# Gate logits summed inside attention, routing by prefix scans, one block at least for every expert

## The reference

```python
# 1: attention, q/k/v of (4, 8, 576, 64), with a learned bias on relative position
scores = q @ k.T / 8 + bias            # bias[h, i, j] from a small MLP of log distances
attn   = softmax(scores);  o = attn @ v
x = o.transpose(0, 2, 1, 3).reshape(2304, 512)        # token = batch * 576 + position
# 2: mixture of experts, top 1 of 8
logits = x @ w_gate                                    # (2304, 8)
expert_idx = argmax(logits);  gate_w = softmax(logits)[expert_idx]
for e in range(8):                                     # an expert without tokens is skipped
    out[mask] = gate_w[mask] * (relu(x[mask] @ w1[e]) @ w2[e])   # w1 512x1024, w2 1024x512
# 3: RMS norm, then silu(xn @ w_gate) * (xn @ w_val) @ w_out, 512 -> 1536 -> 512
```

## Time and profile before

| | |
|---|---|
| runs (us) | 1209.17, 1210.5, 1210.6; median 1210.5 |
| profiled execution (us) | 1211.22, its span 1209.4 |
| PE busy | 1092.7 us, 90% of the span |
| DVE, ACT, POOL busy | 733.8, 515.4, 255.9 us |
| granted PE clock, mean | 0.960 of full |
| DMA | 107.66 MB |

### The profile page before, as it was taken

The page is one execution under the profiler, slowest core; times in us unless marked ns, Lnnn a source line. Parts: engine busy times, 40 slices in busy tenths (PEclk is TensorE's granted clock), DMA queues, the critical chain, the costliest instruction groups (busy, mean ns, idle before and its releaser), DMA issues. The chain is left out here.

```text
span 1209.4 us, 23282 instructions
## 1 busy us (share of the span) xinstructions
PE 1092.7 (90%) x6540; PEld 910.2 (75%) x6541; DVE 733.8 (61%) x1310; ACT 515.4 (43%) x1047; POOL 255.9 (21%) x183
## 2 busy tenths in 40 slices
PE   3969999999996539999999947999999999999998
PEld 1347777777774338878888837999999999999997
DVE  6956656656653654282522227877778778777665
ACT  4967777777662233261522235423222232231211
POOL 3027656655600021020110115320000000000000
PEclk9989999999998759999999987999999999999999
DMA  5574644647305266182111125100010000000000
GB/s 128 231 275 95 173 101 111 171 98 204 80 25 173 97 245 214 43 286 78 35 43 43 42 97 149 60 27 26 0 52 0 26 26 0 26 26 0 27 1 27
DMA packets 71728, 107.66 MB, mean 89 GB/s; under 512 B 28176, under 2 KB 40464, under 8 KB 71696
## 3 DMA queue, kind: packets, MB, share of 16 engines
q1 hardware_dynamic: 68496, 96.78, 26.2%
q0 software_dynamic: 3200, 10.49, 2.8%
HBM read 79.85 MB, written 27.39 MB: 89 GB/s over the span
## 5 line engine op out<-in xcount | busy, mean ns | idle before, releaser
L1438 DVE RECIPROCAL f_eg<-f_eg 128x384 f32<-128x384 f32 x72 | 183.3, 2546 | 0.0
L519 DVE CUSTOM_DVE_ANT_0 a_sc<-a_s_ps,a_bias 128x576 f32<-128x576 f32 x144 | 108.3, 753 | 87.0 <-PE a_s_ps L438 73.3
L1403 ACT ACTIVATE f_eg<-f_g 128x384 f32<-128x384 f32 x72 | 35.4, 492 | 284.5 <-PE f_v L1473 284.4
L584 ACT ACTIVATE a_pr<-a_sc,a_nmax 128x576 f32<-128x576 f32 x144 | 111.9, 777 | 39.3 <-DVE a_nmax L519 35.6
L438 PE MATMUL a_s_ps<-a_khi,a_qs 128*128 128x288 f32 x320 | 103.7, 340 | 9.6 <-PEq L82 8.9
L1473 PE MATMUL f_g<-f_xhi,f_ghi 128*128 (+1 forms) x288 | 99.7, 346 | 5.8 <-DVE f_eg L1442 3.0
L455 PE MATMUL a_t_ps<-ident,a_pr 128*128 128x128 f32 x720 | 103.2, 274 | 1.2 <-ACT a_pr L584 0.5
L1473 PE MATMUL f_g<-f_xlo,f_ghi 128*128 (+1 forms) x288 | 98.4, 342 | 0.0
L1473 PE MATMUL f_g<-f_xhi,f_glo 128*128 (+1 forms) x288 | 98.3, 341 | 0.0
L1473 PE MATMUL f_v<-f_xlo,f_vhi 128*128 (+1 forms) x288 | 97.8, 340 | 0.0
L1473 PE MATMUL f_v<-f_xhi,f_vhi 128*128 (+1 forms) x288 | 97.8, 339 | 0.0
(11 more groups left out here) (225 smaller groups left out, 2462.5 us busy)
## 6 DMA issues: line engine op xcount, KB each, us to landing
e_raw<-ew SPq DMA_DIRECT2D x20, 1024.0 KB, 6.4
bias_ihj<-b_res SPq DMA_DIRECT2D x36, 288.0 KB, 2.1
a_qraw<-q SPq DMA_DIRECT2D x32, 288.0 KB, 5.2
a_kraw<-k SPq DMA_DIRECT2D x32, 288.0 KB, 5.8
a_bias<-bias_ihj SPq DMA_DIRECT2D x16, 576.0 KB, 7.1
y_sorted<-e_out SPq DMA_DIRECT2D x21, 256.0 KB, 2.0
r_x<-x_tokens SPq DMA_DIRECT2D x6, 768.0 KB, 8.4
out<-f_raw SPq DMA_DIRECT2D x18, 256.0 KB, 2.0
```

The lines of the kernel that those rows point to most:

```text
L519: e.tensor_tensor_reduce(sc[:, h, :].rearrange("p (a s) -> p a s", a=2), s_ps[:, h, :, 0:HALF], bias[:, 2 * s + h, :].rearrange("p (c s) - ...
L584: mm = e.activation(pr[:, w, S * h:S * h + S], sc[:, h, :], ACT.Exp, bias=nmax[:, h:h + 1], scale=-1.0, accum_out=sums[:, u, 2 * s + h:2 * ...
L1403: e.activation(eg[:, k % 2, :], g_ps[k % 2][:, 0:CHUNK], ACT.Exp, scale=-1.0).then_inc(s_e, 1)
L1438: e.reciprocal(x, x).then_inc(s_c, 1)
```

## The change

1. In attention `turn_back` becomes a plain f32 matmul with the same left operand, `ot`, and with `xw` on the right: the identity, widened by 8 columns of w_gate for each head. Each tile has 144 columns instead of 128: the turned output and this pair's share of the gate logits. DVE scales both in one instruction and adds the 16 logit columns to `part` (`rt.part`). The last tile has both heads on its diagonal blocks, so `xt` goes and ACT copies its two halves apart.
2. Routing no longer reads x. It adds the two heads' sums, brings the 64-row tails of two batches into one tile with a small matmul (`fold`), and works out the places with two scans. Every expert now has one block at least. The weights are loaded for expert 0, 1, 2, ... in turn, without `If` on the number of used experts.
3. SP loads expert 0's weights at the start of attention. In routing POOL makes the low halves of two chunks and ACT all four high halves. POOL sets routing's constants in attention.
4. The stores of x are more and smaller, and the last two tiles of the output are stored in halves.

```diff
--- before
+++ after
+            e.memset(xw[:, :, :, 64:XW], 0.0).then_inc(s_init, 1)
+            for h in range(2):
+                e.tensor_copy(xw[:, :, h, 0:64], ident[:, 64 * h:64 * h + 64].unsqueeze(1).to_broadcast([P, H // 2, 64]))\
+                    .then_inc(s_init, 1)
...
+            for h in range(2):
+                e.dma_start(xw[64 * h:64 * h + 64, :, h, 64:XW], wg.rearrange("(p h d) e -> h d p e", h=2, d=64)[h])\
+                    .then_inc(s_wg, 16)
...
-                e.dma_start(xd[bass.ds(p % B * S, 2 * P), bass.ds(p // B * P, P)].rearrange("(t p) c -> p t c", p=P),
-                            xp[:, u, 0:2, :]).then_inc(s_st0[u], 16)
+                for t in range(2):
+                    e.dma_start(xd[bass.ds(p % B * S + P * t, P), bass.ds(p // B * P, P)].rearrange("p (h d) -> p h d", h=2),
+                                xp[:, u, t, :, 0:64]).then_inc(s_st0[u], 16)
...
             for i in range(NT, NBLK):
                 e.dma_start(ys[i * P:(i + 1) * P, :], zero[:, :]).then_inc(s_zd, 16)
+            for c in range(4):
+                e.dma_start(ew.raw_of(c), ew.source(c, 0)).then_inc(ew.s_raw[c], 16)
             each_pair(e, pair)
             store_first(NPAIR - 1, 1)
             store_second(NPAIR - 1, 1)
             for u in range(2):
-                e.wait_ge(s_st0[u], sem.at(s_st0[u], 16 * (NPAIR // 2)))
-                e.wait_ge(s_st1[u], sem.at(s_st1[u], 48 * (NPAIR // 2)))
+                e.wait_ge(s_st0[u], sem.at(s_st0[u], 32 * (NPAIR // 2)))
+                e.wait_ge(s_st1[u], sem.at(s_st1[u], 64 * (NPAIR // 2)))
...
             split_q(e, 0, 1)
+            e.memset(ot[64:P, BLK:S], 0.0).then_inc(s_zero, 1)
+            e.wait_ge(s_zero, sem.at(s_zero, 1))
+            e.memset(ot[0:64, S:S + 64], 0.0).then_inc(s_zero, 1)
+            e.wait_ge(s_zero, sem.at(s_zero, 2))
+            rt.constants(e)
             with e.Fori(1, NPAIR // 2) as it:
...
-                    mm = e.transpose(t_ps[1][:, P * t:P + P * t], ot[:, c:c + P], ident[:, :])
+                    mm = e.matmul(t_ps[1][:, 2 * XW * t:2 * XW * (t + 1)], ot[:, c:c + P],
+                                  xw[:, bass.ds(p // B, 1), :, :].rearrange("p a h d -> p (a h d)"), start=True, stop=True)
...
                 if half == 0:
                     e.wait_ge(s_e, sem.at(s_e, p * TPP + TPP))
-                    e.reciprocal(rinv[:, u, :], sums[:, u, :]).then_inc(s_r, 1)
-                    e.wait_ge(s_r, sem.at(s_r, p + 1))
+                    e.reciprocal(rinv[:, u, 0:TPP], sums[:, u, :]).then_inc(s_r, 1)
+                    e.reciprocal(rinv[:, u, TPP:TPP + 1], sums[:, u, TPP - 1:TPP]).then_inc(s_r, 1)
+                    e.wait_ge(s_r, sem.at(s_r, p * 2 + 2))
                 st = (s_st0, s_st1)[half][u]
                 e.wait_ge(s_bk, sem.at(s_bk, p * 2 + half + 1))
-                e.wait_ge(st, sem.at(st, uses * (16, 48)[half]))
-                mm = e.tensor_tensor(xp[:, u, 2 * half:2 * half + 2, :].rearrange("p t (h d) -> p t h d", h=2),
-                                     t_ps[1][:, 0:2 * P].rearrange("p (t h d) -> p t h d", t=2, h=2),
-                                     rinv[:, u, 4 * half:4 * half + 4].rearrange("p (t h) -> p t h", t=2)
-                                     .unsqueeze(3).to_broadcast([P, 2, 2, 64]), ALU.mult)
-                if half:
-                    for h in range(2):
-                        q = slice(64 * h, 64 * h + 64)
-                        mm = e.tensor_scalar(xt[q, u, :], t_ps[1][q, 2 * P + 64 * h:2 * P + 64 * h + 64],
-                                             rinv[q, u, 8:9], None, ALU.mult)
-                mm.then_inc(s_x, 1)
+                e.wait_ge(st, sem.at(st, uses * (32, 64)[half]))
+                e.tensor_tensor(xp[at], t_ps[1][:, 0:2 * XW * n].rearrange("p (t h d) -> p t h d", t=n, h=2),
+                                rinv[:, u, 4 * half:4 * half + 2 * n].rearrange("p (t h) -> p t h", h=2)
+                                .unsqueeze(3).to_broadcast([P, n, 2, XW]), ALU.mult).then_inc(s_x, 1)
+                e.wait_ge(s_x, sem.at(s_x, p * 2 + half + 1))
+                if isinstance(p, int) and p == 0:
+                    e.wait_ge(rt.s_c, sem.at(rt.s_c, 1))
+                part = rt.part[:, bass.ds(p % B, 1), 2 * half:2 * half + n, :].rearrange("p b t (h e) -> p (b t) h e", h=2)
+                e.tensor_tensor(part, part, xp[at + (slice(64, XW),)], ALU.add).then_inc(s_pa, 1)
...
-                mm = e.activation(ot[:, q:q + n], o_ps[:, 0:n], ACT.Copy)
+                mm = e.activation(ot[:, q:q + 2 * P], o_ps[:, 0:2 * P], ACT.Copy)
                 if half:
-                    mm = e.activation(ot[:, S:S + 64], o_ps[:, 2 * P:2 * P + 64], ACT.Copy)
+                    if isinstance(p, int) and p == 0:
+                        e.wait_ge(s_zero, sem.at(s_zero, 2))
+                    for h in range(2):
+                        rows = slice(64 * h, 64 * h + 64)
+                        mm = e.activation(ot[rows, BLK + 64 * h:BLK + 64 * h + 64], o_ps[rows, 2 * P:n], ACT.Copy)
...
         @blk.gpsimd
         def _(e):
+            for c in range(2):
+                ew.lo(e, 0, c)
...
+            e.wait_ge(s_f, sem.at(s_f, 1))
+            e.activation(lg[64:P, tails:NT, :], sides[64:P, :, 1, :], ACT.Copy).then_inc(s_lg, 1)
...
+            e.wait_ge(s_n, sem.at(s_n, 1))
+            do(e.tensor_tensor_scan(flat(pre), rt.ones[:, 0:1].to_broadcast([P, NT * E]), n_ps[:, 0, 0:NT * E], 0.0,
+                                    ALU.mult, ALU.add))
+            start, inc = rt.start, rt.inc
+            do(e.tensor_copy(start[:, 1:E + 1], pre[:, :, NT - 1]))
+            tt(cnt[:, :], start[:, 1:E + 1], start[:, 0:E], ALU.subtract)
+            tt(full[:, :, :], cnt[:, :].unsqueeze(2).to_broadcast([P, E, NT - 1]),
+               thr[:, :].unsqueeze(1).to_broadcast([P, E, NT - 1]), ALU.is_gt)
+            do(e.tensor_reduce(more[:, :], full[:, :, :], AX.X, ALU.add))
+            do(e.tensor_tensor_scan(inc[:, 1:E + 1], rt.ones[:, 0:E], more[:, :], 0.0, ALU.add, ALU.add))
+            do(e.scalar_tensor_tensor(out=delta[:, :], in0=inc[:, 0:E], scalar=float(P), in1=start[:, 0:E],
+                                      op0=ALU.mult, op1=ALU.subtract))
+            tt(pre[:, :, :], pre[:, :, :], over_t(delta[:, :]), ALU.add)
+            e.wait_ge(s_n, sem.at(s_n, 2))
+            tt(flat(pre), n_ps[:, 1, 0:NT * E], flat(pre), ALU.add)
+            tt(at[:, :, :], pre[:, :, :], oh[:, :, :], ALU.mult)
+            do(e.tensor_reduce(dpad[:, :], at[:, :, :].rearrange("p e t -> p t e"), AX.X, ALU.add))
+            do(e.tensor_copy(dest[:, :], dpad[:, :]))
...
 
-                with e.If(runs > r):
-                    ex = e.value_load(tabs[0:1, bass.ds(r, 1)], min_val=0, max_val=E - 1)
-                    for c in range(4):
-                        e.wait_ge(s_w, sem.at(s_w, r * 4 - 3 + c))
-                        sem.apart(e, r * 4 - 3 + c)
-                        e.dma_start(ew.raw_of(c), ew.source(c, ex)).then_inc(s_raw[c], 16)
+                for c in range(4):
+                    e.wait_ge(s_w, sem.at(s_w, r * 4 - 3 + c))
+                    sem.apart(e, r * 4 - 3 + c)
+                    e.dma_start(ew.raw_of(c), ew.source(c, r % E)).then_inc(s_raw[c], 16)
...
-                    load(run + 2)
+                    with e.If(run < E - 2):
+                        load(run + 2)
...
+                if isinstance(c, int) and col >= NT - NT % 4:
+                    for h in range(2):
+                        row = ((col - NT + NT % 4) * 2 + h) * S + 4 * P
+                        e.dma_start(out[row:row + 64, :], ob[64 * h:64 * h + 64, t, :]).then_inc(s_st, 16)
+                else:
+                    e.dma_start(out[bass.ds(col // 4 * S + col % 4 * P, P), :], ob[:, t, :]).then_inc(s_st, 16)
```

More of the change, by code:

```diff
@@ L224, in attention_stage @@
     MIX = 4
+    XW = 64 + E
     HALVES = ((0, 2 * P), (2 * P, S - 2 * P))
@@ L635, in routing_stage @@
+def routing_stage(nc, sem, rt, ew, dest, gate, idx, tabs):
     with ExitStack() as ctx:
@@ L664, in routing_stage @@
+        oh, pre, at = (sb("r_" + n, [P, E, NT]) for n in ("oh", "pre", "at"))
+        cnt, more = sb("r_cnt", [P, E]), sb("r_more", [P, E])
+        full = sb("r_full", [P, E, NT - 1])
+        thr = sb("r_thr", [P, NT - 1])
+        delta = sb("r_delta", [P, E])
+        dpad = sb("r_dpad", [P, NT])
         db_i, db, dq = sb("r_db_i", [P, NT], i32), sb("r_db", [P, NT]), sb("r_dq", [P, NT])
         inb = sb("r_inb", [P, NT, NBLK + 1], f32r)
-        inq = xhi[:, :, :, :].rearrange("p a k s -> p (a k s)")[:, 0:NT * P].rearrange("p (t q) -> p t q", q=P)
@@ L705, in product @@
-        def product(e, g):
-            n = len(groups[g]) * P
-            e.wait_ge(s_lo, sem.at(s_lo, groups[g][-1] + 1))
-            e.wait_ge(s_lt, sem.at(s_lt, g))
-            for k in range(KD):
-                for i, (x, y) in enumerate(((wghi, xhi), (wghi, xlo), (wglo, xhi))):
```

(61 more changed lines are left out.)

323 lines of the change are left out of this document (125 added, 198 removed).

## The result

The changed kernel takes 1254.1 us (median of 4 runs, 1253.1 to 1255.7) against 1209.8 for the kernel before on the same chip: a ratio of 1.037, 95% interval 1.035 to 1.039. The forecast was 1238, with a range up to 1252, so the direction was right and the size 16 us short. The profiled execution has a span of 1253.9 us.

A forecast was written before the change was run, and what follows sets the result against it. PE was taken to bound attention and experts, a chain of dependent steps routing. Experts +42, routing -35, attention +13, early load +7, last stores +0.5 make +27.5 on 1211.2, 1238.7; forecast against the median 1238 us, range 1222 to 1252.

The forecast's parts named there:

- Attention, the turned products: Attention, PE: plain f32 matmuls in place of transposes for five turned tiles, +0.73 us a pair, 11.6 over 16 pairs.
- the small things: Attention, DVE: second reciprocal, 0.03 us longer multiplication, addition of about 0.2, against 0.39 us of slack; 0.1 us a pair left.
- Attention, DVE's chain: Attention: DVE's steps between a pair's two turns, where slack of 0.39 us absorbs all but 0.1 us a pair.
- The early load: Attention: expert 0's four 1 MB loads queue ahead of pair 2's q and k; PE stands 6 us once, +7 in all.
- Routing: Routing stage: the new chain takes 24.3 us in place of 59.4, -35 us (-42 to -30).
- POOL's share: Routing: DVE's small steps wait during POOL's two SBUF subtractions of 4.5 us, 7 us lost (0 to 9).
- Experts: Expert stage: 24 blocks in place of 21, +37.6 us, and +3.9 for first blocks in a row; rounded to +42.
- DVE's late copy and two splits ahead of `e_hlo`: Experts 2 to 5: these delay PE's second product, 7.8 us against 6.5; 1.3 us for each of three blocks, +3.9.
- weights bound the short experts: Rival, experts: weight loads lag, each block from expert 2 to 5 takes 15.5 us, 1247 us in all; 12%.
- Stalls nobody: Rival, attention: q and k don't queue behind the early weight loads, so no 7 us loss, 1231 us; 15%.
- without POOL's waits: Rival, routing: POOL gets in between DVE's steps once or not at all, 8 us less, 1230 us; 12%.
- the blocks are not run: Rival, experts: the loop's count stays 21, empty experts get no block, the 42 us fall away, 1196 us; 3%.

The follow-up runs named there:

- later addition: Changed kernel with the logits' addition moved three slots later, one for all five tiles of a pair, where VectorE and GpSimd stand idle: 1239.9 us, ratio 1.026.
- one-input-from-PSUM kernel: Changed kernel with the logits' addition ahead of the multiplication, one input taken from PSUM and only the other from SBUF: 1242.2 us, ratio 1.027.

## Why the prediction was right or wrong

- **Attention, the turned products: right.** 0.73 us a pair was forecast for PE, 0.83 with the small things; 0.66 is what the later addition leaves over the kernel before.
- **Attention, DVE's chain: this step failed.** The prediction put "an addition of about 0.2" among the small things and left 0.1 us a pair, 1.6 in all. It costs 13.8 us by the times. The addition has two SBUF inputs, it runs beside POOL's split in 13 of the 16 pairs, and it stands ahead of the copies that PE waits for. The one-input-from-PSUM kernel shows the cause, the later addition the size. A quarter of it (3.3 us) comes by a way that DVE's rows don't show: twice PE's longer wait was followed by half clock. What makes it instructive: the same prediction priced the very same wait in routing, from the earlier trace rows, and got it right. It looked for the wait where POOL's instruction was new, and not where DVE's was new and POOL's old.
- **The early load: right step, size short.** One gap ended by POOL's split, as forecast, but 8.2 us and not 6, and with half clock behind it the load costs 11.9 us and not 7. The forecast let the bytes queue at the full 395 GB/s for 10.6 us; POOL starts on pair 2 11.8 us later than before (106.19 against 94.41). The trace has SP itself held up as well, so that q and k are issued up to 94.3; whether this makes the further 1.2 us no run shows (timeline of SP's queue in the changed kernel):

```profile
80.34 4.35 SPq L422 DMA_DIRECT2D e_raw<-ew  x4
84.80 5.05 SPq L251 DMA_DIRECT2D a_qraw<-q  x1
89.89 0.60 SPq L253 DMA_DIRECT2D a_kraw<-k  x1
...
93.73 0.60 SPq L253 DMA_DIRECT2D a_kraw<-k  x1
```

- **Routing: right.** 24.1 us against 24.3, POOL's share 7.5 against 7, the chain without it 16.7 against 17.3.
- **Experts: the number right, one mechanism wrong; that the sum came out is luck.** +42.4 between the copies, 42 forecast. Of this 37.6 are three blocks of 12.52 us. The 4.8 beyond were forecast as 3.9 from DVE's late copy and two splits ahead of `e_hlo`; that wait is not in the trace. They are 2.7 us of weight bytes (the rival "weights bound the short experts", at a third of its 9 us, for the DMA moved 323 to 339 GB/s in these blocks) and 0.7 us for each of three further first blocks, the larger part of it at the block's start, by the low half of a weight. The prediction had read 0.3 us for this from the wait in the earlier trace rows alone; the block copies of before already show 0.7. The first product also comes 2.3 us later behind the border (12.3 against 10.0), since the gather now shares the DMA with weight loads that no wait holds back: with half of their bytes it is 9.6. This was not in the prediction.
- **Rivals.** "Stalls nobody", "without POOL's waits" and "the blocks are not run" are out by rows of the profile after. No rival was a further loss in attention, which is why the range ended at 1252.
- **The sum.** 10.6 (products and small things) + 13.8 (addition) + 11.9 (load) = 36.3 against 34.1 measured in attention, within the 3.5 us that each difference is uncertain by. Against the forecast the addition is 12.2 us more than its 1.6 and the load 4.9 more than its 7: together 17 us, and the miss is 16.
- **The end.** The 2.5 us more in the FFN stretch are not shown to be a loss of the change. From the last block copy to the end it is 499.6 us in the trace of before and 501.5 in that of the changed kernel, but 496.6 and 498.9 in two more traces with the FFN of before and 497.6 to 500.0 in eight with the new one. The two groups differ by 0.6 us on the mean; 0.5 was forecast for the five last stores in place of three.

## What to carry to other kernels

When a change adds a VectorE instruction, ask first how many of its inputs lie in SBUF and what GpSimd does at that moment; if it is an instruction of microseconds, the small step costs up to what is left of it, and everything queued behind pays. Here one PSUM input, or another place in the queue, gave it back (12.0 and 13.8 us). A loop's count is worth more than its body: three blocks without a token cost 42 us, more than the shortened routing gave back (35), so ask of every simplification of an index what it does to the number of passes with the data at hand.
